# Splitting a routed expert's first weights between neighbouring experts, and a reordered routing chain ahead of the first sorted tile

## What is computed

```python
attn_out = _attn_ref(q, k, v, proj)        # 2 x 8 heads, 768 tokens, 64 wide, masked by hashed buckets
x = attn_out.transpose(0, 2, 1, 3).reshape(1536, 512)
# first MoE: all 8 experts on all 1536 tokens, weights P from 8 Sinkhorn steps
for e in range(8):
    out += P[:, e:e + 1] * (np.maximum(x @ w1[e], 0.0) @ w2[e])
# second MoE on that output: one expert for each token
expert_idx = np.argmax(xn @ en.T / tau, axis=1)
for e in range(8):
    mask = expert_idx == e
    out[mask] = gate_w[mask, None] * (np.maximum(x[mask] @ w1[e], 0.0) @ w2[e])
```

## Time and profile before

| | |
|---|---|
| median of 3 runs | 1626.51 us (1625.79 to 1626.74) |
| profiled execution | 1626.99 us, of which the span of the trace is 1625.3 us |
| TensorE matmul busy | 1583.2 us, 97% of the span |
| VectorE, ScalarE, GpSimd busy | 42%, 31%, 20% |
| second MoE's first up matmul | 1387.77 us after the span's start |
| sorted tile 0, 1, 2 | 22.00, 12.43, 18.82 us |

### The profile page before, as it was taken

One profiled execution on the slowest core, in us unless ns is written; L12 is line 12 of the kernel. 1 busy time (PEld: TensorE's weight loads), 2 busy tenths in 40 slices (PEclk: granted clock), 3 DMA queues, 4 the chain that ended last, 5 costly groups with the idle time before them and its releaser, 6 DMA issues.

```text
span 1625.3 us, 21943 instructions
## 1 busy us (share of the span) xinstructions
PE 1583.2 (97%) x7643; PEld 1321.4 (81%) x7644; DVE 687.3 (42%) x1249; ACT 508.6 (31%) x949; POOL 326.8 (20%) x526
## 2 busy tenths in 40 slices
PE   7999999999999999999999999999999999889997
PEld 6999998778888888888888888888888887678886
DVE  5888888342211211212322121121122356787664
ACT  4777777111111101111211111110121233476553
POOL 4455443100300210030030030011003000332333
PEclk8999999999999999999999999999999999899999
DMA  6555554100110110110020010011011121764310
GB/s 152 139 123 115 136 117 152 52 1 0 52 52 1 52 52 0 52 52 0 12 91 0 0 71 33 0 52 52 0 52 52 39 78 67 253 226 150 134 45 24
DMA packets 45592, 110.96 MB, mean 68 GB/s; under 512 B 5926, under 2 KB 7974, under 8 KB 45552
## 3 DMA queue, kind: packets, MB, share of 16 engines
q1 hardware_dynamic: 41248, 100.52, 20.0%
q0 software_dynamic: 3504, 8.14, 1.5%
q10 hardware_dynamic: 800, 1.77, 0.5%
HBM read 81.57 MB, written 8.39 MB: 55 GB/s over the span
## 4 chain that ended last, share of the span: by engine, by line
PE 90%; DVE 4%; issue 2%; POOL 2%; DMA 1%; ACT 1%; DVEq 0%; POOLq 0%; ACTq 0%
PE psum L451 25%; PE psum L453 25%; PE psum L452 25%; PE psum L699 3%; PE psum L688 2%; PE psum L712 2%; PE psum L713 1%; PE psum L689 1%; PE psum L670 1%; DVE row_min L1293 1%; PE psum L993 1%; PE psum L724 1%; DVE pt_lo L1283 1%; DMA w_raw<-in_moe_w_dram 1%; PE psum L816 1%
## 5 line engine op out<-in xcount | busy, mean ns | idle before, releaser
L1150 ACT ACTIVATE h_hi<-psum 128x512 fp32r<-128x512 f32 x192 | 114.7, 598 | 890.8 <-PE psum L453 890.8
L451 PE MATMUL psum<-xt_lo,w_hi 128*128 128x512 f32 x768 | 305.5, 398 | 0.2 <-DVE xt_lo L1386 0.2
L453 PE MATMUL psum<-xt_hi,w_lo 128*128 128x512 f32 x768 | 304.5, 396 | 0.0
L452 PE MATMUL psum<-xt_hi,w_hi 128*128 128x512 f32 x768 | 304.4, 396 | 0.0
L451 PE MATMUL psum<-w_lo,h_hi 128*128 128x512 f32 x768 | 302.0, 393 | 0.0
L453 PE MATMUL psum<-w_hi,h_lo 128*128 128x512 f32 x768 | 299.3, 390 | 0.0
L452 PE MATMUL psum<-w_hi,h_hi 128*128 128x512 f32 x768 | 299.1, 389 | 0.0
L1556 DVE SCALAR_TENSOR_TENSOR h_lo<-psum,h_hi 128x512 fp32r<-128x512 f32 x192 | 132.8, 692 | 368.5 <-ACT h_hi L1150 368.5
L1613 DVE SCALAR_TENSOR_TENSOR tok<-psum,route,tok 128x512 f32<-128x512 f32 x84 | 57.5, 745 | 351.5 <-PE psum L453 351.0
L484 POOL CAST w_hi<-w_raw 128x512 fp32r<-128x512 f32 x64 | 40.0, 625 | 823.5 <-PE psum L453 814.2
L451 PEld LDWEIGHTS psum<-xt_lo,w_hi 128*128 128x128 f32 x768 | 144.6, 188 | 35.1 <-DVE xt_lo L1386 0.4
(11 more groups left out here) (282 smaller groups left out, 2052.5 us busy)
## 6 DMA issues: line engine op xcount, KB each, us to landing
w_raw<-in_moe_w_dram SPq DMA_DIRECT2D x27, 2048.0 KB, 8.2
w_raw_odd<-in_moe_w_dram SPq DMA_DIRECT2D x4, 2048.0 KB
k_hh<-k_hi SPq DMA_DIRECT2D x32, 192.0 KB, 3.0
x_rows<-tok SPq DMA_DIRECT2D x14, 256.0 KB, 2.3
k_raw<-in_k_dram SPq DMA_DIRECT2D x8, 384.0 KB, 3.1
v_raw<-in_v_dram SPq DMA_DIRECT2D x16, 192.0 KB, 3.3
k_b<-k_lo SPq DMA_DIRECT2D x16, 192.0 KB, 3.4
q_raw<-in_q_dram SPq DMA_DIRECT2D x7, 384.0 KB, 3.8
```

The lines of the kernel that those rows point to most:

```text
L451: pe.matmul(acc, a[0], b[1], start=start, stop=False)
L452: pe.matmul(acc, a[0], b[0], start=False, stop=False)
L453: return pe.matmul(acc, a[1], b[0], start=False, stop=stop)
L1150: act.activation(h_s[0][:, f, :], psum[:, f % 4, :], ACT.Relu).then_inc(m1.h_hi, 1)
```

## The change

Six things change together.

1. First weights: there is one home for the split first weights, `w1_s`, for odd and even experts, and two raw buffers, `w1_raw` and one in the first eight token tiles of `tok`. Expert e + 1's are split at the end of expert e, in four pieces of full width, and TensorE waits for each piece in front of its first use. GpSimd has no part in it. The loads are issued in another order: expert 1's pair early, expert 2's second weights at the end of the first MoE, its first weights after the second gather.
2. The small buffers of the routing (`x_row`, `y_row`, `diag`, `hot`, `tab` and others) move from `tok` into columns of `xt`.
3. In the last product, VectorE adds y before `find_cell` instead of behind it; `table_part` is in front of f = 3 instead of f = 2, and the look-up of the first rows (L869) in front of f = 5 instead of f = 3.
4. On TensorE the six identity turns (`keep_busy`) are gone, and the diagonal products stand ahead of the logits of token tile 11 instead of behind the table part; they open the sum in PSUM.
5. VectorE's seven operations from the root to the argument of the exponent move ahead of the wait for the begins. TensorE loads expert 0's end into a register before the slots product and takes expert 0 out of its loop; its first tile is known to be 0.
6. GpSimd copies the indices of a tile before it waits for the tile's y row.

Buffers:

```diff
-    w1_raw2 = place("w1_raw2", [P, KD, FF], F32, [turned + CT * DM * 4])
+    w1_raw_of = [w1_raw, place("w1_raw_odd", [P, KD, FF], F32, [turned])]
-    w2_raw_of = [w2_raw, place("w2_raw_odd", [P, KF, DM], F32, small)]
+    w2_raw_of = [place("w2_raw_even", [P, KF, DM], F32, small), w2_raw]
```

SP's queue:

```diff
         sp.wait_ge(m2.w2_lo, KF)
+        sp.wait_ge(m2.w2_in, 16)
+        sp.dma_start(w2_raw_of[1][:], m2.wb[1]).then_inc(m2.w2_in, 16)
+        sp.wait_ge(s_x_stored, 16 * 2 * CT)
+        sp.wait_ge(s_turned, 2 * CT)
+        sp.wait_ge(s_squares, 2 * CT)
         sp.wait_ge(m2.w1_in, 16)
-        sp.dma_start(w1_raw_b[:], m2.wa[1]).then_inc(m2.w1_in, 16)
+        sp.dma_start(w1_raw_of[1][:], m2.wa[1]).then_inc(m2.w1_in, 16)
         for t in range(2 * CT, HOT):
             store_x(t, s_x_stored)
         for t in range(HOT, TT):
             store_x(t, s_x_last)
         sp.wait_ge(m1.down, CH * E + 1)
-        sp.wait_ge(m2.w2_in, 16)
-        sp.dma_start(w2_raw_of[1][:], m2.wb[1]).then_inc(m2.w2_in, 16)
-        sp.wait_ge(s_x_stored, 16 * HOT)
-        sp.wait_ge(s_x_last, 32)
-        sp.wait_ge(s_squares, TT)
-        sp.wait_ge(s_xrow_t, 1)
-        sp.wait_ge(m2.w1_in, 32)
-        sp.dma_start(w1_raw2[:], m2.wa[2]).then_inc(m2.w1_in, 16)
+        sp.wait_ge(m2.w2_in, 32)
+        sp.dma_start(w2_raw_of[0][:], m2.wb[2]).then_inc(m2.w2_in, 16)
         sp.wait_ge(s_p_ready, 1)
         sp.dma_start(weights_v, per_tok[:, 2, :].rearrange("p (b t) -> p b t", b=B)).then_inc(s_p_stored, 16)
-        sp.wait_ge(s_first_lo, 1)
-        sp.wait_ge(m2.w1_lo, 2)
-        sp.wait_ge(m2.w2_in, 32)
-        sp.dma_start(w2_raw_of[0][:], m2.wb[2]).then_inc(m2.w2_in, 16)
+        sp.wait_ge(s_xrow, 32)
+        sp.wait_ge(m2.w1_lo, KD)
+        sp.wait_ge(m2.w1_in, 32)
+        sp.dma_start(w1_raw_of[0][:], m2.wa[2]).then_inc(m2.w1_in, 16)
...
             sp.dma_start(w2_raw_of[e % 2][:], m2.wb[e]).then_inc(m2.w2_in, 16)
-            sp.wait_ge(m2.w1_lo, e)
+            sp.wait_ge(m2.w1_lo, KD * (e - 1))
             sp.wait_ge(m2.w1_in, 16 * e)
-            sp.dma_start(w1_raw2[:], m2.wa[e]).then_inc(m2.w1_in, 16)
+            sp.dma_start(w1_raw_of[e % 2][:], m2.wa[e]).then_inc(m2.w1_in, 16)
```

GpSimd:

```diff
         def store(i):
-            pool.wait_ge(s_y2, i + 1)
             pool.wait_ge(s_xrow, 16 * i + 32)
             copy(idx_now[:], tab[:, bass.ds(i, 1), :].rearrange("p i c -> p (i c)")).then_inc(s_idx, 1)
             pool.wait_ge(s_idx, i + 1)
+            pool.wait_ge(s_y2, i + 1)
...
-        pool.wait_ge(m2.w1_lo, 1)
-        first_w1_lo(range(2, KD))
```

TensorE:

```diff
-            if t == HOT and f == 3:
+            if t == HOT and f == 5:
                 pe.wait_ge(s_added, 3)
                 pe.matmul(psum[:, 5, 0:1], table[0:CELLS, :], ident[0:CELLS, 0:1], start=True, stop=True).then_inc(s_first, 1)
-            if f == (3 if i == 0 else 2):
+            if f == 3:
...
         turn_token(TT - 1, 0)
-        keep_busy(6)
+        pe.wait_ge(s_diag, 1)
+        pe.wait_ge(s_xrow, 16)
+        for kd in range(KD):
+            pe.matmul(psum[:, 2 + kd, 0:P], x_row[:, kd * P:(kd + 1) * P], diag[:], start=True, stop=False)
         token_logits(TT - 1, 1)
         last_rows(HOT)
...
-        pe.wait_ge(s_diag, 1)
-        pe.wait_ge(s_xrow, 16)
-        for kd in range(KD):
-            pe.matmul(psum[:, 2 + kd, 0:P], x_row[:, kd * P:(kd + 1) * P], diag[:], start=False, stop=False)
         last_rows(TT - 1)
...
+        pe.wait_ge(s_start, 1)
+        first_end = pe.value_load(start_i[0:1, 1:2], min_val=1, max_val=SLOTS)
         pe.wait_ge(s_added, 4)
         pe.wait_ge(s_slot_in, 1)
         pe.matmul(psum[:, 7, 0:COLS], table[0:CELLS, :], slot_of[0:CELLS, :], start=True, stop=True).then_inc(s_slots, 1)
-        pe.wait_ge(s_start, 1)
-        pe.wait_ge(s_first_lo, 1)
...
-                pe.wait_ge(m2.w1_lo, e + 1)
                 pe.wait_ge(s_x_lo, i + 1)
                 for c in range(2):
                     pe.wait_ge(s_relu2, 2 * i + c + 1)
                     for kd in range(KD):
+                        if c == 0:
+                            pe.wait_ge(m2.w1_lo, KD * e + kd + 1)
...
+        tiles2(0, 0, 0, first_end)
```

ScalarE and VectorE, at the end of `expert2(e, u)`, and the new helper of VectorE:

```diff
-            if w1 and u == 0:
-                w1_hi2(e + 2, w1_raw2)
-            if w1 and u == 1:
-                w1_hi2_odd(e + 2, w1_raw2)
+            if more:
+                w1_hi2(e + 1, w1_raw_of[1 - u])
...
-            if w1:
-                dve.wait_ge(m2.w1_lo, e + 2)
-                (w1_lo_even, w1_lo_odd)[u](e + 2, w1_raw2)
+            if more:
+                w1_lo2(e + 1, w1_raw_of[1 - u])
+        def w1_lo2(e, raw, kds=range(KD)):
+            for kd in kds:
+                dve.wait_ge(m2.w1_hi, KD * e + kd + 1)
+                dve.tensor_tensor(w1_s[1][:, kd, :], raw[:, kd, :], w1_s[0][:, kd, :].bitcast(F32),
+                                  ALU.subtract).then_inc(m2.w1_lo, 1)
```

VectorE, in the last product:

```diff
                         choose(2 * CT - 1 + i, 1)
-                        if i < CT - 1:
-                            find_cell(2 * CT - 1 + i, 2)
                         dve.wait_ge(*((s_down_tile, i + 1) if i < CT - 1 else (m1.down, n + 2)))
...
                     if last and c == CH - 1:
-                        if i == 0:
-                            w1_lo_even(0, w1_raw, (1, 2))
-                        if i == 1:
-                            w1_lo_even(0, w1_raw, (3,))
-                            w1_lo_odd(1, w1_raw_b, (0,))
+                        find_cell(2 * CT - 1 + i, 6 if i == CT - 1 else 2)
+                        if i < CT - 1:
+                            w1_lo2(0, w1_raw, (i + 1,))
                         if i == 2:
                             add_part(HOT - 1, 3)
-                            w1_lo_odd(1, w1_raw_b, (1,))
                             first_rows()
```

VectorE, between `find_cell(TT - 1, 6)` and `dve.wait_ge(s_begin, 1)`, moved there from behind the slot table:

```diff
+        dve.wait_ge(s_act_out, 3)
+        root, inv = per_tok[:, 2, :], per_tok[:, 3, :]
+        link(dve.reciprocal(inv, root))
+        link(dve.tensor_tensor(inv, inv, per_tok[:, 0, :], ALU.mult))
+        link(dve.tensor_tensor(inv, inv, root, ALU.add))
+        link(dve.tensor_scalar(inv, inv, 0.5, 1e-6, ALU.mult, ALU.add))
+        link(dve.reciprocal(inv, inv))
+        link(dve.tensor_tensor(g1[:], logit[:], row_bc(4), ALU.subtract))
+        link(dve.tensor_tensor(g1[:], g1[:], row_bc(3), ALU.mult))
+        dve.sem_inc(s_act_in, 1)
```

More of the change, by code:

```diff
@@ L994, in turn_h, with tiles2 @@
             tr.then_inc(s_g_t, 1)
-        def expert2(e, u, more=True):
-            first, end = tile_range(pe, e)
+        def tiles2(e, u, first, end, more=True):
             with pe.Fori(first, end) as i:
-                pe.wait_ge(m2.w1_lo, e + 1)
                 pe.wait_ge(s_x_lo, i + 1)
@@ L1019, in expert2 @@
                 mm.then_inc(s_down2, 1)
+        tiles2(0, 0, 0, first_end)
         with pe.Fori(0, E // 2 - 1) as e2:
-            for u in range(2):
-                expert2(2 * e2 + u, u)
-        for u in range(2):
-            expert2(E - 2 + u, u, more=(u == 0))
+            for u in (1, 0):
+                e = 2 * e2 + 2 - u
+                tiles2(e, u, *tile_range(pe, e))
+        tiles2(E - 1, 1, *tile_range(pe, E - 1), more=False)
     @block.scalar
@@ L1130, in w1_hi2 @@
             for kd in kds:
-                act.copy(w1_s[0][:, kd, :], raw[:, kd, :]).then_inc(m2.w1_hi, 2)
-        def w1_hi2_odd(e, raw, kds=range(KD)):
-            act.wait_ge(m2.w1_in, 16 * e + 16)
-            for kd in kds:
-                for c in range(2):
-                    act.copy(w1_p[1][0][kd][c], raw[:, kd, c * 512:(c + 1) * 512]).then_inc(m2.w1_hi, 1)
+                act.copy(w1_s[0][:, kd, :], raw[:, kd, :]).then_inc(m2.w1_hi, 1)
         def w2_hi2(e, u, raw, fs):
@@ L1204, in y_tile, with expert2 @@
             act.activation(y_row[:], psum[:, 4, :], ACT.Copy, scale=p_now[:, 0:1]).then_inc(s_y2, 1)
-        def expert2(e, u, w1=True, w2=True):
+        def expert2(e, u, more=True):
             first, end = tile_range(act, e)
@@ L1232, in _ @@
                 expert2(2 * e2 + u, u)
-        expert2(E - 2, 0, w1=False)
-        expert2(E - 1, 1, w1=False, w2=False)
+        expert2(E - 2, 0)
+        expert2(E - 1, 1, more=False)
         every = act.value_load(start_i[0:1, E:E + 1], min_val=E, max_val=SLOTS)
@@ L1639, in _ @@
         expert(E - 1, last=True)
-        find_cell(HOT, 6)
         link(dve.memset(p_now[:], 0.0))
         link(dve.tensor_scalar(tab[:, 0, 0:1], tok_id[:, 0:1], 0.0, float(2 * N), ALU.mult, ALU.add))
+        for s, n in ((s_g_lo, 2), (s_relu2, 2), (s_y_free, 1)):
+            dve.sem_inc(s, n)
         choose(TT - 1, 1)
@@ L1705, in second @@
                 def second(*fs):
-                    if w2:
+                    if more:
                         for f in fs:
```

91 lines of the change are left out of this document (24 added, 67 removed).

## The result

The changed kernel takes 1612.53 us (median of 4 runs, 1612.07 to 1612.88); the kernel before took 1626.62 beside it (4 runs, 1625.79 to 1626.86). The ratio is 0.9912, with a 95% interval of 0.9896 to 0.9928. The forecast was 1612.6. The profiled execution took 1612.79 us, with a span of 1611.1 (before: 1626.99, 1625.3), so 14.2 us of span are to be accounted for.

A forecast was written before the change was run, and what follows sets the result against it. TensorE is busy nearly all the time, so only idle or half-rate stretches can be won: 7.0 + 6.4 + 0.7 + 0.5 + 0.5 - 1.2 = 13.9 us off 1626.99, median 0.5 lower, so 1612.6; range 1609.0 to 1618.2.

The forecast's parts named there:

- tile 0: Second MoE's first sorted tile: idle stretch and second half-rate stretch go, first half-rate stretch stays; 15.0 us, 7.0 less.
- tile 2: Third sorted tile: the wait for expert 3's first weights is hidden by the other raw buffer; gain 6.4 us.
- switches and odd experts, tiles 3 to 15: Expert switches in the second MoE: seven cost 1.2 us together, the 0.7 us lost behind odd experts is gained.
- seam, start of tile 0: Between the two MoEs: tile 0's first up matmul comes at 1387.3 instead of 1387.77, 0.5 us gained.
- tail: Last y row to its store: index copy done beforehand, saving 0.2 to 1.1 us, taken as 0.5.
- rival B: Tiles 0 and 2: one of the two big stalls stays, about 6 us of gain lost, 1618.8; chance 0.11.
- The split just in time: Between neighbouring experts' up products: TensorE waits piece by piece, 0 to 0.2 us a switch, 1.2 us for all seven.
- rival C: Seven expert switches: TensorE in effect waits for the whole split, losing 14.7 us instead of 1.2, 1626.1; chance 0.04.
- rival A: Ahead of tile 0: clock falls at about 1376 instead of 1379.8, costing 1.6 to 2.4 us, 1614.6; chance 0.15.
- the moved diagonal product: Ahead of tile 0: its 8 turns leave the last chain; x rows ready 0.4 us earlier, at 1383.1.
- S3 - S2: Sign: time between the first matmuls of tiles 2 and 3, claimed near 12.5 us.
- the y row to the last store: Sign at the kernel's end: this stretch claimed to take about 1 us.

The follow-up runs named there:

- run 1: The kernel before, with GpSimd's four remainders of expert 1's first weights done by VectorE behind the three sums of the routing chain: 1620.05 us.
- run 2: The changed kernel with three idle GpSimd subtractions behind the second gather, writing columns that nothing reads: 1613.22 us.
- run 4: The changed kernel with one raw buffer for first weights instead of two, each load asked for one expert later: 1618.57 us.
- run 11: The changed kernel with expert 3's second-weight load asked for only when the third x-row gather has landed: median 1611.25 us, ratio 0.9908.
- run 7: The changed kernel with VectorE's seven normalisation operations moved back behind the slot table: 1613.21 us.
- run 3: The changed kernel with TensorE waiting for all four pieces of an expert's first weights in front of the first: 1629.83 us.
- run 8: The changed kernel with GpSimd's index copy again behind the wait for the y row: 1613.68 us.
- run 9: The changed kernel with six identity turns back, diagonal product behind the table part, and a one-column VectorE PSUM operation behind each piece of the split: 1611.01 us.
- run 10: The changed kernel with the edits of run 9 and run 11 together: median 1611.60 us, ratio 0.9910.

## Why the prediction was right

| step | forecast | measured |
|---|---|---|
| tile 0 | -7.0 (15.0) | -7.35 (14.65) |
| tile 2 | -6.4 (12.43) | -5.39 (13.43) |
| switches and odd experts, tiles 3 to 15 | +0.5 | -1.48 |
| seam, start of tile 0 | -0.5 | +0.7 |
| tail | -0.5 | -0.6 |
| sum | -13.9 | -14.2, with 0.04 in tile 1 |

**Tile 0.** Right in mechanism and size. GpSimd's hold was the cause (runs 1 and 2), the ReLU came in time, and the second half-rate stretch went. The half-rate stretch that stays is 4.40 us with 10 matmuls, which costs 4.40 - 10 x 0.23 = 2.1 us instead of the 2.6 of the sum; that is most of the 0.35. The ReLU ended at 1394.38 and the turn at 1394.78 waited for nothing, so 0.4 us were to spare instead of 0.8. VectorE was about 1 us later than forecast throughout (ReLU done at 1394.4, not 1393.4), and so was tile 0.

**Tile 2.** The two raw buffers do what the step said (run 4). The 1.0 us that is left is no weight load that ScalarE waits for, as rival B had it, but a wait that the prediction did not look for: a small gather beside a 2 MB load, and a released row behind the gather (gone in run 11, and in runs 2 and 7).

**The split just in time.** The waits came out near the forecast, 1.6 us in six, the longest 0.4 (forecast 1.2 in seven); run 3 shows that rival C's mechanism costs 13.2 in waits, and 17.3 with the clock. The 0.7 us behind odd experts were gained too: tiles 5 and 15 take 12.60 instead of 12.82. The sign of the whole term was nevertheless wrong, because a gain was missing from the sum: odd experts' tiles take 12.29 us instead of 12.42, and there are nine of them in this stretch, 1.2 us. Their up product now reads w1_hi and w1_lo (w_hi and w_lo in the rows), which it streams faster than the old home of the odd weights. Four matmuls of an odd expert after, and of one before:

```profile
1503.43 0.39 PE L444 MATMUL psum<-w_lo,x_hi 128*128 128x512 f32 x1
1503.65 0.39 PE L445 MATMUL psum<-w_hi,x_hi 128*128 128x512 f32 x1
1503.88 0.39 PE L446 MATMUL psum<-w_hi,x_lo 128*128 128x512 f32 x1
1504.11 0.39 PE L444 MATMUL psum<-w_lo,x_hi 128*128 128x512 f32 x1
```

```profile
1516.70 0.39 PE L451 MATMUL psum<-w_odd_lo,x_hi 128*128 128x512 f32 x1
1516.93 0.40 PE L452 MATMUL psum<-xt_hi,x_hi 128*128 128x512 f32 x1
1517.17 0.40 PE L453 MATMUL psum<-xt_hi,x_lo 128*128 128x512 f32 x1
1517.41 0.39 PE L451 MATMUL psum<-w_odd_lo,x_hi 128*128 128x512 f32 x1
```

Start to start that is 0.68 / 3 = 0.227 us after and 0.71 / 3 = 0.237 before. Over all tiles behind 1441 the medians are 0.227 and 0.232 to 0.236; 24 matmuls of an up product by 0.006 are 0.14 us. The down products agree: in both kernels the median is 0.227 to 0.229 where the second weights are in w2_hi and w2_lo, and 0.233 to 0.236 where they are in xt. What about those tensors makes the difference (their place, or what else reads near them) was not tried.

**The seam.** This step failed, by 1.2 us. The 0.7 lost is a seam 1.17 us longer (13.43 against 12.26) less a last product that ended 0.49 earlier, and the latter moves by up to 2.9 us from trace to trace. Two things went wrong. First, the prediction let the clock fall at 1379.8 as before and gave rival A 0.15; it fell at 1376, and did so in five of seven traces of that order. The price of 1.6 to 2.4 us that rival A was given was about right (1.5 to 1.8). Second, the moved diagonal product was to make the x rows ready 0.4 us earlier; with the clock kept, the seam is 11.8 us with it (runs 3 and 8) and 11.3 without it (runs 9 and 10). The order of before with the clock kept takes 11.15 (run 1), so the forecast's 0.5 appears only against the one trace of before whose clock had fallen at 4.3. The waits that the prediction named are there, 0.49 us for the rank (0.75 forecast) and 0.40 for the gather. That the missing filler is what let the clock fall early is likely, not shown.

The total is right partly by luck. Against the forecast tile 0 gave 0.35 more and the switches and odd experts 2.0 more, of which nobody had foreseen 1.2; tile 2 gave 1.0 less and the seam 1.2 less. Errors of 1 to 2 us cancelled to 0.3 in the span.

**Tail.** 0.55 us is the index copy's (run 8), as forecast. Of the signs that the prediction named, two did not come: S3 - S2 is 13.43 and not near 12.5, and the y row to the last store takes 1.59 us and not about 1 (2.15 less the forecast 0.5 would have been 1.65).

## What to carry to other kernels

Filler work in idle time in front of a dependent chain of small matmuls is better kept until its removal has been tried alone: with 0.82 us of it no trace of seven lost the clock early, without it five of seven did, at 1.5 to 1.8 us. Look at several traces before you judge such a seam, since one order showed both cases. When VectorE and GpSimd both work out of SBUF, look at who starts first: a tiny operation or a DMA issue can stand for as long as the other engine's unbroken run, so put work that others wait for ahead of such runs, not 0.03 us into them. A gap in front of an engine's next work can take other work of that engine for almost nothing (VectorE's 2.16 us, run 1). Small transfers that release a row or a buffer should be asked for before large loads, or the loads told to wait until the issue is over.

## What the runs showed of the hardware that was not expected

GpSimd's hold works the other way round too. An indirect gather's issue (0.95 us alone) that begins 0.03 to 0.05 us into VectorE's run of six subtractions from SBUF took 6.62, 6.62 and 6.61 us in three traces and ended each time 0.89 to 0.92 us behind the start of the ReLU that reads PSUM; in four others with the same offset and no pause (runs 3, 4, 8 and 11) it took 2.00 or 2.01, as if it had come in behind the first piece. What decides between the two is open. The Trainium skill's page "SBUF — State Buffer" (section "SBUF: two separate sides") says that descriptors of GpSimd's DMAs can't be written while VectorE holds the shared ports. It says so of operations in a two-port mode, such as copies. The traces agree on the hold, but here it comes with subtractions that have two inputs in SBUF. That page of the Trainium skill also speaks of one instruction at a time, where the 6.6 us here span six and the 5.51 us of the earlier trace rows four.

The same TensorE instructions do not meet the same clock in every trace: half the clock from 1.0 to 1.6 us behind the turn in five traces, from 5.8 us in two, with no idle stretch of TensorE longer than 1.0 us ahead of it. An indirect gather of 128 rows beside a 2 MB load lands some 3.5 us later if the load is asked for before the gather's issue has ended (6.6 to 7.6 us against 3.0 to 4.2). And matmuls of the same shape start every 0.227 us or every 0.234 us, by which tensor they stream.
